# Fused attention, soft MoE and top-2 MoE on one core: the routed experts' setup and tile loop re-ordered, with a second pair of split buffers, a ring of gathered rows, and later weight splits

## The reference

```
x = softmax over the top 32 scores (q k^T / 8) @ v    # 4 batches, 8 heads, 576 rows, width 64
x = soft MoE(x): logits = x @ phi; d = softmax over tokens, c = softmax over slots
    slots = d^T x; slot_out = relu(slots @ w1[e]) @ w2[e];  x = c @ slot_out
x = top-2 MoE(x): noisy = x @ w_gate + log1p(exp(x @ w_noise)) * noise
    per token the 2 best of 8 experts, weights softmax of their logits
    out += weight * (relu(x @ w1[e]) @ w2[e])          # 2304 tokens, D 512, F 1024
```

## Time and profile before

| | us |
|---|---|
| median of 3 runs (lowest, highest) | 1093.74 (1093.58, 1099.24) |
| the profiled execution, its own time | 1097.52 |
| its span in the profile | 1095.7 |
| attention and soft MoE, to the routing | about 735 |
| routing, G, first splits | 735 to 786 |
| tile loop | 786 to 1084 |
| last scatter, last gather, end | 1084 to 1095.7 |

### The profile page before, as it was taken

The page is one execution under the profiler, slowest core; times in us unless marked ns, Lnnn a source line. Parts: engine busy times, 40 slices in busy tenths (PEclk is TensorE's granted clock), DMA queues, the critical chain, the costliest instruction groups (busy, mean ns, idle before and its releaser), DMA issues.

```text
span 1095.7 us, 20890 instructions
## 1 busy us (share of the span) xinstructions
PE 934.0 (85%) x6032; PEld 634.8 (58%) x6032; DVE 808.3 (74%) x1870; ACT 617.3 (56%) x1199; POOL 709.2 (65%) x900
## 2 busy tenths in 40 slices
PE   3888888888888888888888887766699999899995
PEld 1555555555555555555555563223387787788884
DVE  6999999999999999999999964018525443444331
ACT  5788888788888888888888751111414321321110
POOL 2799998999899899899899951003234344344443
PEclk9999999999999999999999998967799999999998
DMA  9910011011011011011101008899524534433332
GB/s 349 401 45 24 24 46 44 0 44 44 0 44 44 0 44 44 0 44 44 39 6 44 0 1 321 351 421 425 225 31 108 117 48 110 108 41 41 41 42 31
DMA packets 21585, 105.12 MB, mean 96 GB/s; under 512 B 2944, under 2 KB 4016, under 8 KB 12464
## 3 DMA queue, kind: packets, MB, share of 16 engines
q1 hardware_dynamic: 13696, 84.54, 19.6%
q0 software_dynamic: 7136, 11.20, 7.8%
q10 hardware_dynamic: 720, 8.98, 2.2%
HBM read 88.37 MB, written 16.07 MB: 95 GB/s over the span
## 4 chain that ended last, share of the span: by engine, by line
PE 37%; DVE 35%; issue 15%; ACT 5%; DMA 5%; DVEq 1%; POOL 1%; SPq 0%; ACTq 0%; POOLq 0%
PE psum L805 12%; DVE arena L996 9%; DVE arena L980 5%; PE psum L810 5%; PE psum L523 5%; PE psum L564 5%; DVE arena L988 5%; DVE arena L1003 4%; ACT arena L829 3%; DVE arena L992 3%; DVE arena L1009 3%; DMA arena<-w_soft 2%; PE psum L794 2%; DMA arena<-xs_rows,arena 2%; DVE w_lo L1207 1%
## 5 line engine op out<-in xcount | busy, mean ns | idle before, releaser
L1289 POOL TENSOR_SCALAR arena<-arena 128x576 bf16<-128x576 f32 x142 | 246.7, 1737 | 46.8 <-DVE arena L1009 25.2
L564 PE MATMUL psum<-arena 128*128 128x130 f32 (+3 forms) x1600 | 226.4, 283 | 0.2 <-ACT arena L855 0.2
L564 PEld LDWEIGHTS psum<-arena 128*128 128x128 f32 (+3 forms) x1600 | 186.1, 179 | 43.1 <-ACT arena L855 13.6
L523 PE MATMUL psum<-arena 64*128 64x288 f32 (+1 forms) x640 | 112.0, 461 | 90.1 <-DVE arena L988 85.7
L1298 POOL TENSOR_TENSOR arena<-arena 128x576 f32<-128x576 f32 x142 | 178.5, 1277 | 0.0
L960 ACT ACTIVATE h_hi<-psum 128x512 fp32r<-128x512 f32 x80 | 43.6, 596 | 215.1 <-PE psum L794 215.1
L836 ACT ACTIVATE arena<-psum,arena 128x576 bf16<-128x576 f32 x144 | 106.6, 740 | 83.3 <-DVE arena L980 83.0
L1237 DVE COPY arena<-psum 128x512 f32 x41 | 28.4, 692 | 164.4 <-PE psum L810 144.3
L805 PE MATMUL psum<-w_hi,h_hi 128*128 128x512 f32 x320 | 134.1, 419 | 5.5 <-DVE arena L1237 2.8
L805 PE MATMUL psum<-w_lo,h_hi 128*128 128x512 f32 x320 | 128.6, 402 | 0.0
L523 PEld LDWEIGHTS psum<-arena 64*128 64x128 f32 (+1 forms) x640 | 44.4, 179 | 138.4 <-DVE arena L988 113.3
(11 more groups left out here) (192 smaller groups left out, 1591.4 us busy)
## 6 DMA issues: line engine op xcount, KB each, us to landing
weights<-w_soft SPq DMA_DIRECT2D x21, 1024.0 KB, 16.2
arena<-qkv SPq DMA_DIRECT2D x15, 1189.0 KB, 5.2
weights<-w_top SPq DMA_DIRECT2D x12, 1024.0 KB, 27.1
arena<-w_soft SPq DMA_DIRECT2D x11, 1024.0 KB, 11.8
weights<-w_top SPq DMA_DIRECT2D x3, 2048.0 KB, 18.7
weights<-w_top ACTq DMA_DIRECT2D x3, 2048.0 KB, 7.7
out<-arena SPq DMA_DIRECT2D x1, 4864.0 KB, 18.2
arena<-w_top SPq DMA_DIRECT2D x4, 1024.0 KB, 27.6
```

The lines of the kernel that those rows point to most:

```text
L523: last = nc.tensor.matmul(bank(2 * (t % 2) + x, SH)[q0:q0 + rows, :], qT[u][half, w * P + q0:w * P + q0 + rows], kT[u][half, h * SH:(h + 1 ...
L564: last = nc.tensor.matmul(o_place(n, k)[0:rows, :], wT[0:kr, t % 2, kc, q0:q0 + rows], v_, start=(kc == 0), stop=(kc == KC - 1))
L1289: nc.gpsimd.tensor_scalar(keep[t % 2], s_sb[t % S_SLOTS], kth_sb[:, t % S_SLOTS:t % S_SLOTS + 1], None, ALU.is_ge) \
```

## The change

1. **G earlier.** `g_group` becomes `g_part(g, x)`, a half group. Both halves of group 0 are put ahead of the two rank matmuls, the first half of group 1 behind them, the second half behind the list matmuls. A second pair of split buffers (`gq2_hi`, `gq2_lo`) lies where the scaled rows were before they went to the table, so ScalarE waits for `tabled` before it fills it; the wait of group 1 for the stacks of group 0 is gone.
2. **Stacks in two pairs of banks.** All stacks use banks (3, 4) and (0, 5) in turn. Stacks 6 and 7 move from ahead of the loop to behind experts 1 and 2; ScalarE copies both halves of G 4 to 7 out behind experts 0 to 3 (`g_out(e + 4, 2)`).
3. **Ring of gathered rows.** `x_in` becomes `x_ring` of two slots, and ScalarE copies a slot four times side by side into `x_cur` (`x_copy`); TensorE turns it with one transpose instead of four narrow matmuls. GpSimd gathers four tiles ahead (`AHEAD`), each gather waits for the landing of the one before, and the gather's list column is now fetched apart from the scatter's, between the scatter and the gather.
4. **Splits later, and rows first.** w2 of expert e+1 (second half) and e+2 (first half) are split on ScalarE behind expert e, both halves of e+1 on VectorE, instead of two or three experts ahead. TensorE waits for them inside the tile, at the half that needs them. The very first half goes to GpSimd (`w_lo_first`).
5. **Table of bounds.** `tab` is written before the one-hot tables, so all engines can read it sooner; VectorE reads one bound per expert.

```diff
-        G_BANKS = [(3, 4), (0, 5), (3, 4), (0, 5), (1, 2), (6, 7), (3, 4), (0, 5)]
+        G_BANKS = [(3, 4), (0, 5)] * 4
+        G_SPLIT = [(gq_hi, gq_lo), (gq2_hi, gq2_lo)]
...
+            g_part(0, 0)
+            g_part(0, 1)
             pe.wait_ge(st, 9)
...
-            g_group(0)
+            g_part(1, 0)
+            pe.wait_ge(rt_ready, 1)
+            bounds = tile_bounds(pe)
...
+            g_part(1, 1)
             pe.wait_ge(pick_set, 1)
             for e in range(4):
                 g_stack(e)
-            g_group(1)
-            for e in range(4, E):
+            def f_trans(n):
+                pe.wait_ge(x_c, n + 1)
+                nc.tensor.transpose(bank(B_X, P), x_cur, ident).then_inc(f_t, 1)
...
+            f_trans(0)
+            for e in range(4, 6):
                 g_stack(e)
+            pe.wait_ge(w_lo_first, 1)
             for e in range(E):
-                pe.wait_ge(w_lo, 2 * e + 2)
...
                         if f % 4 == 0:
+                            if 2 * e + f // 4 > 0:
+                                pe.wait_ge(w_lo, 2 * e + f // 4)
...
+                if e in (1, 2):
+                    g_stack(e + 5)
```

ScalarE ahead of the loop, and behind each expert:

```diff
+            act.wait_ge(tabled, 16)
+            g_high(1, 0)
+            g_high(1, 1)
+            w2_high(0, 0)
+            g_out(0)
+            g_out(1)
+            x_copy(0, x_ring[:, 0:SL])
+            g_out(2)
+            g_out(3)
             c_high(1)
+            w2_high(0, 1)
+            x_copy(1, x_ring[:, SL:2 * SL])
+            w2_high(1, 0)
...
                     c_high(i + 2)
-                if e == 0:
-                    g_out(6)
-                    g_out(7)
-                    w2_high(2)
-                if e < E - 3:
-                    w2_high(e + 3)
+                    x_copy(i + 2, x_ring[:, bass.ds((i + 2) % 2 * SL, SL)])
+                if e < E - 1:
+                    w2_high(e + 1, 1)
+                if e < E - 2:
+                    w2_high(e + 2, 0)
+                if e < 4:
+                    g_out(e + 4, 2)
```

VectorE behind each expert, and GpSimd:

```diff
-                if e < E - 2:
-                    w2_low(e + 2)
+                if e < E - 1:
+                    w2_low(e + 1, 0)
+                    w2_low(e + 1, 1)
+                    bounds.append(tile_bound(dve, e + 2))
...
+            for n in range(2):
+                fetch(nowx[n], n, 0, idx_x, n)
+                if n > 0:
+                    pool.wait_ge(x_ready, 16 * n)
+                gather(n)
+            pool.wait_ge(w_hi, 1)
+            nc.gpsimd.tensor_tensor(w2_lo[0][:, 0:FC // 2, :], w2t_of(0)[:, 0:FC // 2, :],
+                                    w2_hi[0][:, 0:FC // 2, :].bitcast(F32), ALU.subtract).then_inc(w_lo_first, 1)
...
-                    hold(pool, f_t, 2 * i + k + 3)
+                    hold(pool, x_c, 2 * i + k + AHEAD - 1)
+                    fetch(nowx[k], 2 * i + k + AHEAD, 0, idx_x, 2 * i + k + AHEAD)
+                    hold(pool, x_ready, 32 * i + 16 * k + 16 * AHEAD)
                     gather(k)
```

More of the change, by code:

```diff
@@ L63 @@
 ROWS = 2 * N
-COLS = TILES + 3
+AHEAD = 4
+COLS = TILES + AHEAD
 PICKS = 2 * TT
@@ L136, in build @@
         list_i = list_f.bitcast(I32).rearrange("p (n v) -> p n v", v=2)
-        now = [take(2).bitcast(I32) for _ in range(2)]
+        nowx, nowo = [[take(1).bitcast(I32) for _ in range(2)] for _ in range(2)]
         tab = take(32).bitcast(I32)
@@ L197, in build @@
         cw = logit
+        x_cur = logit_f[:, 0:P]
         cT = cT_f.rearrange("p (b q) -> p b q", b=5)
@@ L315, in build @@
         f_h, f_hc, f_lo = sem("f_h"), sem("f_hc"), sem("f_lo")
-        w_hi, w_lo = sem("w2_hi"), sem("w2_lo")
+        w_hi, w_lo, w_lo_first = sem("w2_hi"), sem("w2_lo"), sem("w2_lo_first")
         f_y, f_yc = sem("f_y"), sem("f_yc")
@@ L722, in _, with g_part, g_stack @@
             last.then_inc(sp_, 1)
+            def g_part(g, x):
+                for s in range(4):
+                    pe.wait_ge(w1t_in[4 * g + s][x], 16)
+                for c in range(DC):
+                    for s in range(4):
+                        last = nc.tensor.matmul(bank(G_GROUP[g][x])[32 * s:32 * s + 32, :], soT[:, c, :],
+                                                w1t_of(4 * g + s, x, c), start=(c == 0), stop=(c == DC - 1),
+                                                skip_group_check=True)
+                last.then_inc(g_ps, 1)
+            def g_stack(e):
+                pe.wait_ge(g_lo, 2 * (e // 4) + 2)
+                if e >= 2:
+                    pe.wait_ge(g_ev[0], e - 1)
+                    pe.wait_ge(g_ev[1], e - 1)
+                for x in range(2):
+                    for n, part_ in enumerate(G_SPLIT[e // 4]):
+                        first = (1 - n) * SL
+                        last = nc.tensor.matmul(bank(G_BANKS[e][x]), pick[:, e % 4, first:first + P],
+                                                part_[:, x * BANK:(x + 1) * BANK], start=(n == 0), stop=(n == 1))
+                    last.then_inc(g_rep, 1)
+            g_part(0, 0)
+            g_part(0, 1)
             pe.wait_ge(st, 9)
@@ L812, in _ @@
                     last.then_inc(f_y, 1)
-            tl = bounds[E]
-            for n in range(2):
-                hold(pe, x_ready, 16 * tl + 16 * n + 32)
-                pe.sem_inc(f_t, 1)
+                if e in (1, 2):
+                    g_stack(e + 5)
         @block.scalar
```

177 lines of the change are left out of this document (70 added, 107 removed).

## The result

| | before | after |
|---|---|---|
| median of the runs compared (lowest, highest) | 1095.38 (1093.58, 1099.24) | 1077.83 (1076.19, 1079.51) |
| ratio, 95% interval | | 0.9832 (0.981 to 0.9854) |
| profiled execution: own time, span | 1097.52, 1095.7 | 1079.51, 1077.7 |
| first of the big matmuls (L805, now L812) | 791.60 | 783.58 |
| from the first tile's to the 40th's | 286.28 | 275.34 |

The change makes the kernel 1.7% faster; I had forecast 1080.2, from a median of 1093.74 before. The spans differ by 18.0 us: 8.0 before the loop, 10.9 in it, and 1.0 given back at the end.

The account below looks back on a forecast made before the run. TensorE's own time bounds a steady tile (6.99 us), leaving gaps and the loop's start: -8.1 start, -6.7 gaps, +1.3 end make -13.5, from 1093.74 to 1080.2 us. Own range 1073 to 1086; with two rivals 1073 to 1089.

Parts of the forecast that it names:

- The start: Ahead of the loop: first L805 at about 783.5 instead of 791.60, 8.1 us earlier; bounds 4.3 and 12.6.
- rival 1: Start won by half: rank matmuls at low clock or GpSimd's w2_lo half held up; 1084 to 1086 us, chance 0.14.
- The loop: Gaps between first and 40th tile fall from 13.7 to 7.0 us, 6.7 gained; bounds 3 and 13.
- The cold first tile: Loop's first tile still starts on a cold array: 6.24 - 3.93 = 2.3 us of gap.
- VectorE at 7 borders: Two w2_lo halves plus one bound read make y_out about 0.3 us late at each border: 2.1 us.
- ScalarE, 0.8 us forecast: Behind experts 0 to 3, x_copy may wait for its gather among splits and G copies: 0.2 us x 4.
- Stacks 6 and 7: Moved into the loop: 2.0 us of matmuls, some 0.7 covering lateness at the same border, so 1.3 us.
- A 2 MB load beside the gather: In the loop, such a load slows a gather; mostly absorbed by a ring two tiles ahead: 0.5 us.
- The end: Last gather issued behind a list copy, 1.3 us later after the last scatter: +1.3 us; bounds 0 and 2.
- Rival 2: At every border, VectorE's w2_lo halves hold up GpSimd's list copy and gather: 7 us, 1087, chance 0.10.
- Rival 3: GpSimd becomes the loop's bound: 7.5 us a step, 20 us less what is gained ahead, about 1098; chance 0.06.
- Rival 4: Both early gathers take 6.3 us behind 2 MB loads; loop starts at 791 to 794; 1088 to 1093 us, chance 0.08.

Follow-up runs that it names:

- the repeat: The changed kernel run once more, unedited, as the measure for its variants: median 1077.62 us, ratio 0.9828 to the kernel before.
- rank first: Changed kernel with the two rank matmuls put between the halves of group 0 instead of behind both: median 1076.99 us, ratio 0.9817 to the kernel before.
- gathers apart: Changed kernel with a semaphore of its own for the first gather, so the second needn't wait for its landing: median 1073.96 us, ratio 0.9792.
- first half on VectorE: Changed kernel with the first half of w2_lo of expert 0 on VectorE instead of GpSimd: median 1077.82 us, ratio 0.9804 to the kernel before.
- even splits: Kernel before, with ScalarE splitting one expert's w2 behind each expert, not two behind the first: median 1096.91 us, ratio 0.9994.
- the ring alone: Kernel before plus only the two-slot ring, x_copy, one transpose and gathers four tiles ahead: median 1089.76 us, ratio 0.9915.
- both edits: Changed kernel with rank matmuls between group 0's halves and a separate semaphore for the first gather: median 1074.07 us, ratio 0.9792.
- stacks first: Changed kernel with both edits, plus stacks 0 and 1 with their copies out ahead of group 1's second half: median 1072.88 us, ratio 0.9774.
- staggered splits alone: Kernel before with only the change's later, half-by-half w2 splits and TensorE's waits for them, no ring: median 1092.54 us, ratio 0.9942.

## Why the prediction was right

**The start, -8.1 against -8.0.** Right in sum, and by the mechanism named: two gathers in a row, 6.18 and 5.97 us for the 6.3 taken, the first from 767.92 (said: 767.5), and x_copy, w2_high, h_hi behind them. That the size came out to 0.1 us is partly luck. Inside it two errors cancelled in this trace. The half group took 6.50 us, as rival 1 had it, and put the rank matmuls at 747.83 instead of 746.0. But from there to the gather it took 20.1 us, where it had taken 21.9: the rank matmuls ran warm, and VectorE's scan was no longer beside GpSimd's work (0.46 us for 0.86, and 0.18 for 0.95, L1153 and L1157 before). I had counted only the first of these. In the repeat neither error is as large: the half took 3.64 us, the rank matmuls stood at 746.16, the first gather came at 766.20, and the loop started 8.9 us earlier. The run with the rank first shows VectorE's part from the other side. The lower bound of this term was worked out wrongly: at the low clock the half takes 3.5 x 6.24 / 3.93 = 5.6 us, which puts the rank matmuls at 748.1, 4.2 us late and not 5.5, and the gain at 6.0 and not 4.3. I said that the gathers would set the start; what I did not see is that the wait between them was needless, worth 2.7 us in the trace and 3.7 in the median.

**The loop, -6.7 against -10.9.** This term was mis-sized: gaps of 7.0 forecast, 2.9 measured, just under the lower bound of 3. By its items:
- The cold first tile: 2.04 us more than a steady one, for 2.3.
- VectorE at 7 borders, 2.1 us forecast: nothing. The bound that it reads costs no visible time; y_out stands 6.99 us behind its predecessor. The step that failed is the 0.26 us for a register load. It came from a row in which the loads followed short work (2.33 us for 9); here VectorE's sequencer reads the bound at 816.14 (L388), while the first half (815.13 to 817.42) is still running.
- ScalarE, 0.8 us forecast: 0.22, at the border behind expert 0 only, where the w2 load's issue (0.38 us at 819.51) stood ahead of h_hi. x_copy didn't wait where the splits are; where it did (5.03 us at 932.40), no split was behind it.
- Stacks 6 and 7: 0.88 us each, 1.8 for 1.3. I had counted lateness that they would cover; there was none.
- A 2 MB load beside the gather, 0.5 forecast: nothing in the first trace, 0.3 us in the repeat, 0.4 with the rank first and with the gathers apart, 0.7 with the first half on VectorE, all at the same tile. The mechanism is the one named.
- Eight tiles, four each of experts 3 and 7, take 6.84 to 6.89 us instead of 6.985, which offsets 1.0 us; six do so in the kernel before. What sets them apart stays open.

**The end, +1.3 against +1.0.** Right: the last gather starts 2.79 us after the last scatter (said: 3.2), where it was 1.90 before.

**The rivals.** Rival 2's mechanism is there and its price is not: list copy and gather are held up by about 1.3 and 1.0 us at each border, and at borders without a 2 MB load that costs nothing, with the ring or without it; where a tile was late (7.30 us in the repeat), the landing of 8.24 us beside such a load was the larger part. The Trainium skill (SBUF — State Buffer, Who interferes with whom) says that a VectorE instruction with two SBUF inputs contends with a GpSimd instruction that reads SBUF, and that the one issued first holds the other up for its whole length. The trace agrees both ways: 2.05 and 2.10 us on GpSimd beside VectorE's halves, and 5.32 instead of 2.29 us on VectorE (777.39) behind GpSimd's tensor-tensor, which ended at 780.55. Rival 3, GpSimd as the bound, came near its condition: a step of 7.53 us at the borders. But there is one such step per expert, and not forty; the other steps fit into a tile. Rival 4's condition, two landings of 6.3 us, was also the forecast's own, so it could not tell the two apart; it fell with the landing of the second gather, at 780.9: both landings were as slow as it had them (6.18 and 5.97 us), and the loop started 8 us earlier than it gave.

**The range.** 1073 to 1086 us is narrower than the bounds of the terms add up to: 12.6 + 10.7 us gained would give 1070.4, and 4.3 + 0.7 gained with 2 lost 1090.7.

## What to carry to other kernels

A hand-over that waits for "all landed so far" puts two transfers in series, at 6 us each here; a semaphore for the first one took 3.7 us off the median at no cost. Where several engines hand work over at the same border, an edit on one of them can move the gap to the next without shrinking it: with even splits ScalarE's gap behind expert 0 came back as VectorE's wait for ScalarE at every border. A gap counted in one trace is one execution's: for the ring alone the trace gave 4.6 us less and the median 8.3, so set the profiled execution's own time beside the median before adding parts up. A delay that runs beside a wait is not its cause until the landing is looked up: the held-up gather landed in time, and the 2 MB load beside the next one made the tile late. And before an instruction is moved earlier, look which engine will then work beside it.

## What the runs showed of the hardware that was not expected

- A register load that ran on VectorE's sequencer beside a 2.29 us instruction cost no visible time; 9 of them after a short operation left 2.33 us.
- VectorE's scan of 144 columns took 0.46 us alone and 1.30 beside GpSimd's tensor-tensor; a tensor_scalar of 8 columns 0.18 and 0.94.
- The same half group of matmuls took 6.50 us after 3.48 us of idle time (mean granted clock 0.55, so mostly the lower of the two levels, 1.2 GHz) and 3.64 after 1.92 (1.00, all at 2.4 GHz; the changed kernel, twice); group 1's second half took 5.37 after 2.23 us (0.68) and 3.7 after 0.23 (1.00; both edits, then stacks first). Between these pairs the longer idle time has the lower clock, but the idle time alone does not sort all of them: group 1's first half ran at a mean of 0.72 after 2.76 us (changed kernel, 751.27), and the rank matmuls with the half behind them at 1.00 after 3.12 us (rank first, 743.58).
- A gather of 128 rows under saturated loads landed in 6.0 to 7.4 us in these runs, against 3.5 in the loop. In the loop, issued between 1 us before and 5 us behind a 2 MB load of w2, it took 4.4 to 8.6 us; the last three of the loop took 4.2 to 5.7 without one (kernel before, and staggered splits alone).
- A gather whose issue took 2.1 to 2.2 us beside VectorE's halves landed 3.4 to 3.8 us after its start where no such load was near. Those issued in 1.1 us mostly took 2.4 to 3.3 us with the ring and 3.2 to 3.8 without it, so the hold-up added 1 us at most.
